# Two 64-row matmuls in place of two half-filled full passes, in the expert layers of an fp32 kernel

## What is computed

```python
# y = gated linear attention over q, k, v (2 x 8 heads x 768 steps x 40), laid out as x: 1536 tokens x 320
x = leaky(x @ w_in) @ w_out                     # 320 -> 2048 -> 320, leaky(h) = max(0.01 h, h)
logits = x @ w_gate                             # 1536 x 8
P = np.exp(logits - logits.max())
for _ in range(8):                              # normalised by rows, then by columns, eight times
    P /= P.sum(1, keepdims=True) + 1e-09
    P /= P.sum(0, keepdims=True) + 1e-09
    P *= N / E
for e in range(E):                              # E = 8 experts
    h = np.maximum(x @ w1[e], 0.0)              # 320 -> 1024
    ye = h @ w2[e]                              # 1024 -> 320
    out += P[:, e:e + 1] * ye
```

## Time and the profile before

| | |
|---|---|
| three runs, us | 1112.46, 1112.94, 1113.39 (median 1112.94) |
| profiled execution, span, us | 1112.4 (the execution's own time; nothing beside the span is listed) |
| TensorE matmuls busy | 983.9 us, 88% |
| TensorE weight loads busy | 867.8 us, 78% |
| VectorE, ScalarE, GpSimd busy | 449.3, 297.1, 142.1 us |
| chain that ended last | PE 72%, issue 13%, DVE 7%, POOL 6% |

### The profile page before, as it was taken

The page is one execution under the profiler, slowest core; times in us unless marked ns, Lnnn a source line. Parts: engine busy times, 40 slices in busy tenths (PEclk is TensorE's granted clock), DMA queues, the critical chain, the costliest instruction groups (busy, mean ns, idle before and its releaser), DMA issues.

```text
span 1112.4 us, 15930 instructions
## 1 busy us (share of the span) xinstructions
PE 983.9 (88%) x5493; PEld 867.8 (78%) x5493; DVE 449.3 (40%) x769; ACT 297.1 (27%) x571; POOL 142.1 (13%) x263
## 2 busy tenths in 40 slices
PE   6899999999999995000799999999999999999998
PEld 4788888888879995000689999889999989998997
DVE  8999855546623320000342342342332432332222
ACT  5454434334522212000021221221221221221111
POOL 6456100000003222233100000000000000000000
PEclk8899999999999998555799999999999999999999
DMA  9753300300300300000030030020012003000000
GB/s 153 121 73 47 104 1 1 104 0 0 104 1 1 104 1 0 0 0 0 0 104 1 0 104 1 1 71 33 0 43 61 0 1 103 0 0 0 24 24 24
DMA packets 67164, 39.14 MB, mean 35 GB/s; under 512 B 51488, under 2 KB 63264, under 8 KB 67136
## 3 DMA queue, kind: packets, MB, share of 16 engines
q1 hardware_dynamic: 67136, 38.78, 15.2%
HBM read 36.81 MB, written 1.97 MB: 35 GB/s over the span
## 4 chain that ended last, share of the span: by engine, by line
PE 72%; issue 13%; DVE 7%; POOL 6%; POOLq 1%; DVEq 0%; ACT 0%; ACTq 0%
PE psA L1120 35%; PE psB L1158 8%; PE psB L1160 8%; PE psB L1159 8%; PE psB L1136 2%; PE psB L1138 2%; PE psB L1137 2%; POOL rs L523 2%; DVE sg L849 2%; POOL csum L532 1%; PE psB L1143 1%; PE psB L1142 1%; DVE ug L826 1%; DVE ws L796 1%; PE psA L1008 1%
## 5 line engine op out<-in xcount | busy, mean ns | idle before, releaser
L1158 PE MATMUL psB<-w2s,gh 128*128 128x320 f32 x768 | 238.5, 311 | 103.6 <-DVE gl L933 103.6
L695 ACT ACTIVATE gh<-psA 128x512 fp32r<-128x512 f32 x192 | 114.4, 598 | 619.4 <-PE psA L1120 619.4
L933 DVE SCALAR_TENSOR_TENSOR gl<-psA,gh 128x512 fp32r<-128x512 f32 x192 | 132.4, 691 | 334.7 <-ACT gh L695 334.6
L1159 PE MATMUL psB<-w2s,gh 128*128 128x320 f32 x768 | 238.0, 310 | 0.0
L1160 PE MATMUL psB<-w2s,gl 128*128 128x320 f32 x768 | 237.9, 310 | 0.0
L1158 PEld LDWEIGHTS psB<-w2s,gh 128*128 128x128 f32 x768 | 144.7, 188 | 109.4 <-DVE acc L957 102.5
L1120 PE MATMUL psA<-xl,w1h 128*128 (+1 forms) x480 | 189.5, 395 | 0.0
L1120 PE MATMUL psA<-xh,w1h 128*128 (+1 forms) x480 | 189.3, 394 | 0.0
L1120 PE MATMUL psA<-xh,w1l 128*128 (+1 forms) x480 | 189.1, 394 | 0.0
L1159 PEld LDWEIGHTS psB<-w2s,gh 128*128 128x128 f32 x768 | 144.8, 189 | 5.3
L1160 PEld LDWEIGHTS psB<-w2s,gl 128*128 128x128 f32 x768 | 145.0, 189 | 0.0
(11 more groups left out here) (186 smaller groups left out, 999.7 us busy)
## 6 DMA issues: line engine op xcount, KB each, us to landing
raw<-in_moe_w_dram SPq DMA_DIRECT2D x16, 640.0 KB, 8.2
raw<-in_moe_w_dram SPq DMA_DIRECT2D x8, 1024.0 KB, 5.3
raw<-in_moe_w_dram SPq DMA_DIRECT2D x16, 256.0 KB, 6.3
raw<-in_moe_w_out_dram SPq DMA_DIRECT2D x4, 640.0 KB, 10.8
raw<-in_moe_w_in_dram SPq DMA_DIRECT2D x2, 1024.0 KB, 6.3
qs<-in_q_dram SPq DMA_DIRECT2D x12, 160.0 KB, 3.2
ks<-in_k_dram SPq DMA_DIRECT2D x12, 160.0 KB, 3.9
vz<-in_v_dram SPq DMA_DIRECT2D x24, 80.0 KB, 3.8
```

Source lines behind the costliest of these rows:

```text
L695: act.activation(gh[:, f % RING, :], h_ps[:, f % RING, :], ACT.Relu).then_inc(ghi_ok, 1)
L933: dve.scalar_tensor_tensor(out=gl[:, f % RING, :], in0=h_ps[:, f % RING, :], scalar=0.0, in1=gh[:, f % RING, :].bitcast(F32), op0=ALU.max, ...
L1158: pe.matmul(bank, gh[:, slot, cols], W2S[par][:, f, 0, :], start=first, stop=False)
L1159: pe.matmul(bank, gh[:, slot, cols], W2S[par][:, f, 1, :], start=False, stop=False)
```

## The change

In the experts, and only there, hidden tiles are made in pairs. Each tile of a pair gets its first seven passes as before. The eighth is a matmul of 64 rows: for the first tile the high part in partitions 0 to 63 of xr with rows 0 to 63 of W1L, for the second the same high part in partitions 64 to 127 of a new tile, xr2, with rows 64 to 127 of W1L. The two follow each other and write different banks. (Low x low falls away.) Each has its own increment of h_ready, so that both tiles of a pair are announced at its end.

ScalarE makes one more copy of 64 x 512 for each of the three blocks, into xr2, ahead of that into xr. On TensorE, expert_run takes the place of run_block in the experts: pair (0, 1), pair (2, 3), outputs of 0 and 1, pair (4, 5), outputs of 2 and 3, pair (6, 7), outputs of 4 to 7. The loop over token blocks is written out. Ahead of the logits stands pair (0, 1), behind them pair (2, 3). The programs of VectorE, GpSimd and the DMA queues are not touched.

```diff
+        xr2 = sb("xr2", [P, T], F32R)
...
                     act.wait_ge(x2_step, tb + 1)
+                    act.copy(xr2[DR:P, tok], ysum[0:DR, KT, tok])
                     act.copy(xr[0:DR, tok], ysum[0:DR, KT, tok]).then_inc(x2hi, 1)
...
+            def hidden_pair(par, tb, u, f):
+
+                tok = slice(tb * TB, (tb + 1) * TB)
+                for k in range(2):
+                    fs = slice((f + k) * P, (f + k + 1) * P)
+                    bank = h_ps[:, (f + k) % RING, :]
+                    pe.wait_ge(g_ready, u + k + 1)
+                    for t in range(KT):
+                        pe.matmul(bank, W1H[par][:, t, fs], xh[:, t, tok], start=t == 0, stop=False)
+                        pe.matmul(bank, W1L[par][:, t, fs], xh[:, t, tok], start=False, stop=False)
+                        pe.matmul(bank, W1H[par][:, t, fs], xl[:, t, tok], start=False, stop=False)
+                    pe.matmul(bank, W1H[par][:, KT, fs], xr[:, tok], start=False, stop=False)
+                for k, (rows, rest_hi) in enumerate(((slice(0, DR), xr), (slice(DR, P), xr2))):
+                    fs = slice((f + k) * P, (f + k + 1) * P)
+                    pe.matmul(h_ps[:, (f + k) % RING, :], W1L[par][rows, KT, fs], rest_hi[rows, tok],
+                              start=False, stop=True).then_inc(h_ready, 1)
...
-            for f in range(LAG):
-                hidden(0, 0, HALVES * NTB * NF + f, f)
+            hidden_pair(0, 0, HALVES * NTB * NF, 0)
...
-            hidden(0, 0, HALVES * NTB * NF + LAG, LAG)
+            hidden_pair(0, 0, HALVES * NTB * NF + 2, 2)
...
-            run_block(0, HALVES, 0, expert_out, 0, done=LAG + 1)
-            with pe.Fori(1, NTB) as tb:
-                run_block(0, HALVES, tb, expert_out, tb)
-            with pe.Fori(0, NTB) as tb:
-                run_block(1, HALVES + 1, tb, expert_out, NTB + tb)
+            def expert_run(par, s, tb, blk, done=0):
+                pe.wait_ge(w_ready, PIECES * (s + 1))
+                for f in range(0, NF + 2, 2):
+                    u = (s * NTB + tb) * NF + f
+                    if done <= f < NF:
+                        hidden_pair(par, tb, u, f)
+                    if f >= 2:
+                        for k in (2, 1):
+                            expert_out(par, blk, u - k, f - k).then_inc(g_used, 1)
+
+            for tb in range(NTB):
+                expert_run(0, HALVES, tb, tb, done=4 if tb == 0 else 0)
+            for tb in range(NTB):
+                expert_run(1, HALVES + 1, tb, NTB + tb)
             with pe.Fori(1, E // 2) as it:
                 for par in range(2):
                     s = 2 * it + HALVES + par
-                    with pe.Fori(0, NTB) as tb:
-                        run_block(par, s, tb, expert_out, (s - HALVES) * NTB + tb)
+                    for tb in range(NTB):
+                        expert_run(par, s, tb, (s - HALVES) * NTB + tb)
```

## The result

The changed kernel takes 1138.35 us (median of 4 runs, 1137.37 to 1138.74) against 1112.71 us before (4 runs): a ratio of 1.0234, 95% interval 1.022 to 1.0249, so 25.6 us slower. The profiled execution took 1137.37 us with a span of 1135.4. Some 2.0 us lie outside the span, and later runs of the kernel before show 1.8 there, so that this part plays no role. Behind the end of TensorE's long wait traces vary less: all_unrolled and early_logits run the same code there and take 583.7 and 583.6 us, quads and quads_early 566.2 and 566.4. The most that is seen in the first passes behind the wait is 1.0 us, between all_unrolled and the change.

What follows compares the result with a forecast made beforehand. Bound by TensorE to the gate logits, then GpSimd, up to 535.48 us, and by TensorE alone behind it. Pairs +19.0 and logits +2.1 make +21.1 us on the 1112.9 median: 1134 us, range 1123 to 1146.

Steps and rivals of the forecast that it cites:

- the term of the pairs: Expert pairs on TensorE's path: each costs +0.244 us, 78 pairs +19.0 us.
- a lag near 0.10 us: Pairs' 64-row passes: drain and overlap, second starting 0.10 us behind the first; the forecast of 1134 us, chance 0.46.
- The overlap without lag: Rival for the pairs: drain, both 64-row passes starting together, +11.2 us for the pairs, 1126 us, chance 0.18.
- A change of rows lets the array run empty: TensorE at 128 to 64 rows and back: next weight load starts 0.32 us behind the last pass, where 0 is usual.
- the upper bound given (0.376): Most a pair costs: second 64-row pass streams after the first, +0.376 us a pair, +29.3 us in all.
- The lag of the second pass: Within a pair, the second 64-row pass starts 0.10 us behind the first, as loads follow one another by 0.10 us.
- my lower bound of 0.144: Least a pair costs: no lag between its 64-row passes, +0.144 us a pair, +11.2 us in all.
- Unrolling at nothing: TensorE's written-out token loops: nothing gained, and the longer instruction stream with two taken branches left also priced at nothing.
- The logits: Path to the gates: ScalarE's lgt copies fall behind the second pair's activation, so the normalisation starts 2.1 us later.
- My signs for it: Profile signs of the later gates: copy of pg near 318, TensorE resuming near 537.6.
- What hides the rest: ScalarE and VectorE work behind pairs: under 4 us for two tiles, covered by TensorE's output passes and next pair; priced at nothing.

Runs made afterwards that it cites:

- all_unrolled: The changed kernel with its last loop, over pairs of experts, written out as well, 64-row passes kept: 1125.64 us, 1.0121 of the kernel before.
- early_logits: all_unrolled, but ScalarE and VectorE do two tiles ahead of the logits in place of three: 1123.24 us, 1.0113 of the kernel before.
- quads: The changed kernel with all loops written out, four 64-row passes in a row for four tiles, acc addition later: 1106.54 us, 0.9964 of the kernel before.
- quads_early: quads with two tiles in place of three ahead of the logits on ScalarE and VectorE: 1104.18 us, 0.9933 of the kernel before.
- apart: all_unrolled, but each tile's 64-row pass stands right behind its own seven full passes: 1175.19 us, 1.0579 of the kernel before.
- one_half: all_unrolled, but the second 64-row pass of a pair takes the same rows as the first: 1148.23 us, 1.0318 of the kernel before.
- full_loops: The changed kernel with full eighth passes and token loops kept as hardware loops, pair order only: 1112.82 us, 1.0003 of the kernel before.
- full_unrolled: The changed kernel with every eighth pass full again, pair order and token loops written out kept: 1124.76 us, 1.0111 of the kernel before.

## Why the prediction was right, and where it was not

The direction and the range held, and so did the drain at a change of rows. That the sum is so near, 1134 against 1138.35, is luck: the term of the pairs was 8.2 us too large, and the jumps, which take 11.7 us and so nearly half of what the change costs, stood in it at nothing. The case that I had most faith in (a lag near 0.10 us, 0.46) is not the one that came. The overlap without lag is, which I gave 0.18 and priced at 1126 us; the change without its jumps, all_unrolled, takes 1125.64. With the lag that I took and the jumps as they are, the sum would have been about 1146, the edge of my range.

- *A change of rows lets the array run empty: right.* Load 0.32 us late going over, again coming back, 0.10 us from load to streaming, all as read from the earlier trace rows. apart and one_half show it from both sides: 0.38 us for a lone 64-row pass in the place of a full one, 0.39 for a pair in series (30.3 / 78), the upper bound given (0.376).
- *The lag of the second pass: the mis-sized term.* I took 0.10 us "because the array takes weights one load after another in every row I have". All those rows were loads into the same rows of the array. Loads into different rows start together (x2 in one row, 0.19 us), and the passes within 0.01 us. A pair costs 0.155 us by the rows at 654 and 0.156 by the stretches of all_unrolled and full_loops, near my lower bound of 0.144 and not 0.244. The term is 12.2 us, less 1.4 that the order of tiles gives back, 10.8 us and not 19.0. The figure of the Trainium skill that I set beside it ("TensorE: Matmul & The Clock Gate", Part 3: some 4 ns between starts on different row groups) agrees with the trace, which has 3 or 4 ns, and for this term the sum by it was the better one.
- *Unrolling at nothing: wrong.* I reasoned from the missing gaps at the block edges of before. Those jumps go back over one block, 160 passes, or over two such loops; the new one goes back over six, 960. It happens twice and costs 11.7 us by the rows, partly as a wait and partly because the passes behind it run at the lower clock level (granted 0.50) for 2.5 to 5.3 us; where the wait is gone, in all_unrolled, the passes of the same time (766 to 770) have a granted clock of 1.00. full_unrolled against full_loops (11.9 us) and the change against all_unrolled (12.7 us) show it twice. The Trainium skill has the rule, in "Runtime: NRT & Kernel Launch", Instruction fetch mechanics: a taken branch whose target is outside the window held must first fetch it. The trace agrees with the rule: each hole holds one packet of 16 KB on q8, and the jumps of the kernel before move none. A packet by itself makes no hole, as the 25 in all_unrolled's stretch show. That the whole wait is this fetch is not shown, only that it comes with the jump and holds one.
- *The logits: right in kind, +1.7 for +2.1 us.* The pairs there are shorter than I had them, in part by the same lag. My signs for it missed: pg was copied at 316.91 and not near 318, and TensorE resumed at 534.85 and not near 537.6, since this execution was quicker ahead of the pairs and in GpSimd's stage. The later start shows in quads_early against quads, 2.4 us.
- *What hides the rest: right.* VectorE and ScalarE release TensorE nowhere behind the long wait, and full_loops (1.0003) shows the pair order free.

The sum as measured: 10.8 + 11.7 + 1.7 = 24.2 us of the 25.6. The stretch by itself is 23.6 us longer: 10.8 + 11.7, and 1.0 us right behind the long wait, where the passes of all_unrolled come back to the upper clock level sooner than those of the change (granted clock of the first 8 us 0.81 against 0.67). The kernel before has 0.66 there, so at an equal clock the 10.8 would be nearer 12. The rest is within what GpSimd's stage varies by: from the copy of pg to the first addition into acc, traces of these kernels show 214.3 (quads) to 219.0 us (one_half), with the same instructions of GpSimd.

## What to carry to other kernels

Passes on half of the array's rows do run side by side, but going over and back costs about 0.39 us here beyond the passes themselves, so put at least four of them between two changes, or leave the full pass. When code is written out inside a loop, look at how long the loop's body gets: a jump back that was free over 160 or 320 passes cost 5 to 7 us each time over 960, clock included, and writing out the last loop as well removed it. Where between the two it begins was not tested. Work taken ahead of an unavoidable wait is a gain in full, and a copy in another engine's queue can lose it again.

## What the runs showed that I had not expected

- Weight loads for different rows of the array start together: two loads in 0.19 us, four passes of 64 rows in 0.73 us.
- Changes in the number of output columns cost nothing (24 passes with 8 columns in 5.6 us), changes in the number of rows cost about 0.2 us each.
- The same two waits at a jump (1.2 and 3.0 us from start to start) are followed by passes at 0.43 us in place of 0.23 for 2.5 us in one case and 5.3 us in the other. Why they differ stays open.
- Full passes run at 0.227 us for a dozen in a row in some blocks and at 0.231 to 0.232 in others, in the change (651.61 to 654.33) and in the kernel before alike (590.60 to 593.32). Their mean in the stretch is 0.231 us in both, so it has no part in the price of a pair. Why they vary stays open.
